# Loading the second chunk in two parts and moving the first angle product ahead of the second chunk's results

## The reference

```python
for t in range(S):                       # retention
    state = gamma * state + k[:, :, t] ⊗ v[:, :, t]
    y[:, :, t] = scale * q[:, :, t] @ state
# x = y as (batch, token, channel)
theta = x @ w_theta                      # the angles
zr, zi = x * cos(theta), x * sin(theta)
y = w_tok_r @ zr + w_tok_i @ zi          # token mixing
u = x + y;  x2 = u + relu(u @ w_ch)
h = relu(x2ᵀ @ w_tok1) @ w_tok2;  u = x2 + hᵀ
out = u + relu(u @ w_ch1) @ w_ch2
```

## Time and profile before

| | us |
|---|---|
| median of 3 runs | 424.56 |
| profiled execution | 424.39 |
| its span | 422.5 |
| PE busy | 415.8 (98% of the span) |
| DVE busy | 305.6 (72%) |
| ACT busy | 179.0 (42%) |
| POOL busy | 115.4 (27%) |

### The profile page before, as it was taken

The page is one execution under the profiler, slowest core; times in us unless marked ns, Lnnn a source line. Parts: engine busy times, 40 slices in busy tenths (PEclk is TensorE's granted clock), DMA queues, the critical chain, the costliest instruction groups (busy, mean ns, idle before and its releaser), DMA issues.

```text
span 422.5 us, 7038 instructions
## 1 busy us (share of the span) xinstructions
PE 415.8 (98%) x2820; PEld 394.7 (93%) x2820; DVE 305.6 (72%) x428; ACT 179.0 (42%) x273; POOL 115.4 (27%) x107
## 2 busy tenths in 40 slices
PE   7999999999999999999999999999999999999997
PEld 4778787899999999999988999999999999999997
DVE  3799998879999998234432895566546899999941
ACT  1354654754455456311221368134236733355500
POOL 1322341000210002999270008199350100000000
PEclk9999999999999999999999999999999999999999
DMA  8975797620395112101100330001022975520121
GB/s 300 423 264 189 297 229 197 113 73 28 117 194 187 52 50 67 37 0 51 50 22 29 149 150 1 2 0 51 0 76 79 349 171 129 96 76 19 57 81 70
DMA packets 12479, 47.78 MB, mean 113 GB/s; under 512 B 1184, under 2 KB 3360, under 8 KB 10656
## 3 DMA queue, kind: packets, MB, share of 16 engines
q1 hardware_dynamic: 9488, 33.03, 20.9%
q0 software_dynamic: 2816, 14.16, 14.7%
q10 hardware_dynamic: 144, 0.14, 0.2%
HBM read 41.04 MB, written 6.29 MB: 112 GB/s over the span
## 4 chain that ended last, share of the span: by engine, by line
PE 96%; DVE 2%; DMA 1%; issue 0%; DVEq 0%
PE ps L1242 86%; PE ps L1259 3%; PE ps L1299 3%; PE ps L1313 2%; PE ps L1390 1%; PE ps L1273 1%; PE ps L1289 1%; DMA qkv_in<-qkv 1%; DVE prob L892 1%; DVE w_sq L876 0%; DVE x_lo L916 0%; DVE res L911 0%; DVE total L1177 0%; DVE state L902 0%; DVEq L899 0%
## 5 line engine op out<-in xcount | busy, mean ns | idle before, releaser
L1242 PE MATMUL ps<-tw,zs 128*128 128x384 f32 x504 | 88.1, 335 | 0.0
L1242 PEld LDWEIGHTS ps<-tw,zs 128*128 128x128 f32 x504 | 87.3, 188 | 0.1
L1242 PE MATMUL ps<-h_ops_c,w_even 128*128 128x384 f32 x288 | 50.6, 334 | 0.0
L1242 PEld LDWEIGHTS ps<-h_ops_c,w_even 128*128 128x128 f32 x288 | 50.0, 188 | 0.0
L1242 PE MATMUL ps<-u_a,w 128*128 128x384 f32 x210 | 39.9, 334 | 0.0
L1242 PE MATMUL ps<-u_b,w 128*128 128x384 f32 x210 | 39.9, 334 | 0.0
L696 ACT ACTIVATE zs<-z 128x768 fp32r<-128x768 f32 x28 | 23.7, 847 | 37.2 <-PE ps L1242 37.2
L1242 PEld LDWEIGHTS ps<-u_b,w 128*128 128x128 f32 x210 | 36.7, 188 | 0.0
L1242 PEld LDWEIGHTS ps<-u_a,w 128*128 128x128 f32 x210 | 36.7, 188 | 0.0
L1242 PE MATMUL ps<-ut,w_sq 128*128 128x384 f32 x192 | 35.5, 338 | 0.0
L1242 PEld LDWEIGHTS ps<-ut,w_sq 128*128 128x128 f32 x192 | 33.0, 188 | 0.0
(11 more groups left out here) (142 smaller groups left out, 784.9 us busy)
## 6 DMA issues: line engine op xcount, KB each, us to landing
qkv_in<-qkv SPq DMA_DIRECT2D x11, 1024.0 KB, 6.8
raw<-tok POOLq DMA_DIRECT2D x7, 1152.0 KB, 9.0
stage<-weights SPq DMA_DIRECT2D x11, 512.0 KB, 3.4
w_raw<-ch POOLq DMA_DIRECT2D x6, 768.0 KB, 7.1
cols_out<-res SPq DMA_DIRECT2D x2, 1536.0 KB, 5.9
total<-cols_out SPq DMA_DIRECT2D x4, 768.0 KB, 11.1
cols_out<-total SPq DMA_DIRECT2D x16, 192.0 KB, 1.8
raw<-tok SPq DMA_DIRECT2D x6, 384.0 KB, 6.9
```

The costliest lines, as they stand in the source:

```text
L1242: mm = pe.matmul(dst, left(l), right(r), start=first and n == 0, stop=last and n == 2, skip_group_check=True)
```

## The change

Four edits, all at the start of the program. SP sends for the first half of chunk 1 (queries and keys in columns) with a semaphore of its own, then for both halves of w_theta, and then for the second half of chunk 1. ACT makes the high part of w_theta's first half before that of chunk 0. DVE makes the low parts of w_theta and of chunk 0 before it masks the scores of chunk 1. PE does `theta(0)` before `outputs(1)`. No instruction is added or dropped on PE, DVE, ACT and POOL; SP has one transfer more, of the same bytes in all.

```diff
+        second_qk_in = sem("second_qk_in")
@@ sync
-            load_chunk(1)
+            sp.dma_start(qkv_in[:, 1, 0:2 * DM], qkv[1, :, 0:2 * DM]).then_inc(second_qk_in, 16)
             sp.wait_ge(first_qk_in, 16)
             for i in range(2):
                 at = slice(i * THETA_HALF, (i + 1) * THETA_HALF)
                 sp.dma_start(raw[:, 0, at], theta_w[:, at]).then_inc(theta_in[i], 16)
+            sp.dma_start(qkv_in[:, 1, 2 * DM:4 * DM], qkv[1, :, 2 * DM:4 * DM]).then_inc(chunk_in[1], 16)
@@ scalar
             for g in range(NG + 2):
+                if g == 0:
+                    theta_high(0)
                 if g < NG:
                     x_high(g)
                 if g == 0:
-                    for i in range(2):
-                        theta_high(i)
+                    theta_high(1)
@@ vector
-                if g + 1 < NG:
-                    weigh(g + 1)
-                if g < NG:
-                    x_low(g)
                 if g == 0:
-                    for i in range(2):
-                        theta_low(i)
+                    theta_low(0)
+                    x_low(0)
+                    theta_low(1)
+                    weigh(1)
+                else:
+                    if g + 1 < NG:
+                        weigh(g + 1)
+                    if g < NG:
+                        x_low(g)
@@ tensor, scores(g)
-                if g:
+                if g == 1:
+                    pe.wait_ge(second_qk_in, 16)
+                    pe.wait_ge(prob_ready, 1)
+                elif g:
@@ tensor, the loop
                 if g and g % NC < NC - 1:
                     keys_values(g)
+                if g == 1:
+                    theta(0)
                 outputs(g)
                 if g == 0:
                     keys_values(0)
-                if g == 1:
-                    theta(0)
```

## The result

The changed kernel took 430.69 us (median of 6 runs, 429.93 to 431.77) against 424.59 us for the kernel before. The ratio is 1.0133, with a 95% interval of 1.0116 to 1.0151. I had forecast 426.2 us, no change that can be told, with a range of up to 428.3; it is 1.3% slower, and outside the range. The profiled execution took 431.27 us with a span of 429.4 us, against 422.5 before: 6.9 us more.

What follows compares the result with a forecast made beforehand. PE, busy 405.3 of 407.8 us behind the head, was taken as the bound. +2.69 for the wait on the keys and −0.99 for waits falling away gave +1.70: 426.1 profiled, 426.2 median, range 425.2 to 428.3.

Steps and rivals of the forecast that it cites:

- a new wait replaces the one removed: On PE: `keys_values(1)` waits for the keys until 13.68 instead of 10.99, +2.69; waits that fall away give −0.99.
- the part of the chain through DVE: DVE masks chunk 1's scores after the low parts, taking 1.22 us out of the chain to `theta(0)`; buys nothing.
- Where the half lands: On SP's DMA queue: the second half of chunk 1 lands at 12.2, some 2.6 us later than before.
- the shortened cover: On the DMA queue: chunk 3 issued after 12.2, not about 10, but chunk 2 fills it until 14.8; costed nothing.
- Rival (c): On the DMA queue: the half chunk lands at 13 or after, between chunk 2's; +2.5 to +3.0, 427.3; 7 in 100.
- The clock: a rival: On PE: its clock falls in the new 2.6 us gap, slowing 3.55 us of work; +2.2, 428.4; 15 in 100.
- the likeliest case: Half chunk lands at 12.2, `scores(2)` starts 1.70 us later; median 426.2, own range 425.6 to 427.0; 70 in 100.
- The range: For the whole kernel's time: 425.2 to 428.3 us, with under 2 in 10 left outside.
- The early end: The half lands so early that `keys_values(1)` doesn't wait; `theta(0)` starts at 13.0; +0.4, 425.0; 6 in 100.

Runs made afterwards that it cites:

- with and without fillers: The changed kernel with five idle 128x512 matmuls on PE ahead of `keys_values(1)`, beside the changed kernel itself; with them 428.97 us, ratio to before 1.0097.
- without SyncE's wait: The changed kernel without SP's wait for the first half of chunk 0 ahead of sending w_theta; 428.56 us, ratio to before 1.0084.
- the halves in order: The changed kernel with the second half of chunk 1 sent right behind its first, ahead of w_theta; 427.54 us, ratio to before 1.0059.
- both causes taken away: The changed kernel without SP's wait ahead of w_theta and with three idle 128x512 matmuls ahead of `keys_values(1)`; 427.63 us, ratio to before 1.0065.
- fillers in the order alone: The changed kernel with chunk 1 loaded whole ahead of w_theta and two idle 128x512 matmuls ahead of `theta(0)`; 426.45 us, ratio to before 1.0033.

## Why the prediction was wrong

- **That a new wait replaces the one removed: right.** POOL released PE ahead of `keys_values(1)`, everything stood behind it, and the part of the chain through DVE bought nothing. PE stayed full behind the head, and no new gap appeared later. Neither sign that I had set down for being wrong came: `keys_values(1)` did not start before 12.5, and PE waited for nothing beyond 25 us.
- **Where the half lands: this step failed.** I wrote that "by the bytes ahead of them" the halves of w_theta land at 9.6 and 11.1 and the half of chunk 1 at 12.2. It landed at 14.7. The count of bytes was right: sent early enough, the same transfers landed at 10.0, 11.2 and 12.5. What the count left out is when each was sent. Before, chunk 1 kept the queue full until 9.6 and w_theta was sent at 5.27. Now half a chunk keeps it full only until 8.5, and the first of the 16 DMA engines took up w_theta about 2.3 us after it was sent. There the queue ran at 262 GB/s. The 16 parts of the first half of w_theta came in from 9.4 to 12.1, where before they came within 0.7 us. The early parts were on the predicted time; the semaphore counts the last. I had costed the shortened cover at nothing, because the DMA share read 1.05 from 10 us on in the kernel before. That row was of a queue that had been filled early. The term was mis-sized by 2.42 us (5.11 against 2.69). Rival (c), at 7 in 100, had the sign that came, `k_dec` at 13 or later, but neither the size nor the cause: it put the half behind parts of chunk 2, at 13.5 at the latest, while both halves of w_theta, which stand ahead of it, were late already (12.1 and 13.4).
- **The clock: a rival, at 15 in 100, that came true.** My price for it was 2.2 us, at a ratio near the 1.54 of the first score matmuls; the 3.55 us of work took 6.33 us, a ratio of 1.78, and the price was 2.78 by the sum of the rows and 2.7 between the two profiles with and without fillers. In the profile with a wait of 3.1 us it fell as well, so the 426.2 of the likeliest case needed a clock that in these runs did not hold. I had leaned on one gap of 1.4 us which left the clock alone. Other executions show it fallen after a gap of 1.5 us. The Trainium skill, "TensorE: Matmul & The Clock Gate", section "Why this matters for your kernels", warns of idle gaps between bursts of matmuls; the traces agree, with the clock at 0.50 behind waits of 5.5 and 3.1 us (and of 2.4 and 1.5 us in two others), and I should have given the rule more than 15.
- **The range** took the two as alternatives. Both come from one delay, and add up: for the profiled execution I had 426.1, and 426.1 + 2.4 + 2.8 = 431.3, where it took 431.27. The median, 430.69, is 0.6 lower.
- **The early end** (+0.4) never came about: with chunk 1 whole and ahead, w_theta lands at 11.1 and not at 9.6, so the order alone costs 1.5 us at the full clock.

## What to carry to other kernels

Before a transfer is split or moved, look at two times for each one behind it: when it is sent, and when the queue reaches it. In these kernels the bytes ahead gave its landing only where it was sent well before it was reached; shortening what stood ahead of it made it later. And price a new wait on TensorE with the clock that it may cost, in the same case and not as an alternative, because the work behind the long wait ran at half the clock here and took 1.8 times as long; then ask what instruction stands first behind the late operand, and whether it could stand behind work that needs none.

## What the runs showed of the hardware that I had not expected

- A transfer that the queue reached soon after it was sent ran unevenly over the 16 engines: 262 and 235 GB/s in two such stretches, against 408 and 444 in the kernel before, and a last part 2.4 and 2.3 us late. Counted from sending it to the landing of the first of the 16 parts of the transfer ahead of it, that was 2.6 us in the changed kernel and 1.3 us in the kernel with chunk 1 sent later. At 3.8 us (the kernel before) and 5.1 us (without SyncE's wait) the parts landed within 0.7 us; at 3.7 us (the halves in order) within 1.1 us, and 0.5 us late. What happens inside stays open.
- TensorE's clock fell to 0.50 in or just behind waits as short as 1.53 us in some profiles (the halves in order, both causes taken away, fillers in the order alone) and not in others (1.52 us in the changed kernel, 1.56 us with chunk 1 sent later). In the three where it fell, the score matmuls of chunk 0, just ahead of the wait, had all been fast (1.16 us in all); in the seven profiles where they took longer (1.21 to 1.90 us) the wait was 1.41 to 1.48 us, and the clock held. What decides between those with fast scores and a wait of about 1.5 us stays open. That a clock fallen in this wait makes the runs of the kernel before near 426 is argued from their mean clock of 0.996; no trace of such a run was kept.
- The column of the granted clock reads 1.00 over the first matmuls, though they are slow (418 ns a score matmul against 271). The trace of the kernel before has its first clock record at 6.5 us. Durations, not the column, tell the level at the start of a trace.
